# Three chained layers in one kernel: the tile's transposes cut into 64-row halves, and moved to other slots

## The reference, cut to what matters

```python
# x: (2, 4096, 192), weight_gen: (2, 4096, 8 heads, 7 taps)
w = softmax(weight_gen, axis=-1)
x1 = causal 7-tap convolution of x, head h (24 channels) weighted by w[:, :, h, :]
h = np.maximum(x1 @ w_in, 0.0)      # (8192, 192) @ (192, 2048)
x2 = h * h @ w_out                  # (8192, 2048) @ (2048, 192)
h = x2 @ w_in2
out = h * np.cos(h) @ w_out2
```

## Time and profile before

| | |
|---|---|
| median of 3 runs | 1298.72 us (1298.04 to 1299.22) |
| the profiled execution's own time | 1302.44 us |
| its span on the core | 1300.7 us |
| PE / DVE / ACT / POOL busy | 96% / 74% / 63% / 29% |
| mean granted clock of TensorE | 0.984 of full |

### The profile page before, as it was taken

How to read it: one execution, slowest core, us unless ns; L and a number is a source line. 1 busy time by engine, 2 the same in 40 slices (tenths; PEclk the granted TensorE clock), 3 DMA queues, 4 the chain that set the end, 5 groups by cost and what they waited for, 6 DMA issues and landing times.

```text
span 1300.7 us, 24802 instructions
## 1 busy us (share of the span) xinstructions
PE 1244.6 (96%) x9728; PEld 1076.9 (83%) x9728; DVE 965.2 (74%) x1439; ACT 822.8 (63%) x1487; POOL 372.4 (29%) x245
## 2 busy tenths in 40 slices
PE   3898999999999999999999999999999999999997
PEld 2555789898898979889897988989798998989755
DVE  7866777777877777787777778777777778777664
ACT  2477666666666666666666666666666666666654
POOL 3635560512406060330606042150604124000000
PEclk9887999999999999999999999999999999999998
DMA  5230000000001000000100000000100000000000
GB/s 164 63 104 12 32 31 1 14 31 14 31 1 43 2 14 31 14 31 2 44 1 14 31 13 32 13 31 1 39 6 14 31 13 1 2 13 2 13 1 24
DMA packets 13235, 31.72 MB, mean 24 GB/s; under 512 B 1348, under 2 KB 8770, under 8 KB 12992
## 3 DMA queue, kind: packets, MB, share of 16 engines
q1 hardware_dynamic: 13120, 30.14, 7.0%
HBM read 23.84 MB, written 6.29 MB: 23 GB/s over the span
## 4 chain that ended last, share of the span: by engine, by line
PE 82%; DVE 10%; issue 3%; ACT 3%; DMA 1%; SPq 0%; DVEq 0%; ACTq 0%
PE y L390 38%; PE h L390 38%; DVE h L814 2%; PE h L444 2%; DVE turns L797 1%; DVE h L793 1%; PE h L454 1%; DVE g_lo L826 1%; DVE g_lo L830 1%; ACT relu L655 1%; DVE y_part L811 1%; DVE xa_lo L818 1%; ACT turns L682 1%; ACT g_hi L705 1%; PE h L451 1%
## 5 line engine op out<-in xcount | busy, mean ns | idle before, releaser
L390 PE MATMUL y<-g_hi,wo 64*128 64x512 f32 x2820 | 557.2, 394 | 0.0
L390 PE MATMUL y<-g_lo,wo 64*128 64x512 f32 x1880 | 398.9, 391 | 0.0
L347 POOL TENSOR_TENSOR tap<-xc,gen 128x768 f32<-128x768 f32 x105 | 166.4, 1591 | 654.2 <-PE h L444 638.8
L390 PEld LDWEIGHTS y<-g_hi,wo 64*128 64x128 f32 x2820 | 300.7, 184 | 36.6 <-DVE xa_lo L818 3.3
L682 ACT ACTIVATE turns<-turns 128x512 f32<-128x512 f32 x256 | 161.8, 632 | 209.2 <-DVE turns L797 208.8
L814 DVE TENSOR_TENSOR h<-h,turns 128x512 f32<-128x512 f32 x256 | 179.1, 699 | 144.4 <-ACT turns L682 139.5
L793 DVE SCALAR_TENSOR_TENSOR h<-h,relu 128x512 f32<-128x512 f32 x256 | 178.7, 698 | 114.7 <-ACT relu L655 111.5
L655 ACT ACTIVATE relu<-h 128x512 f32<-128x512 f32 x256 | 152.9, 597 | 135.0 <-PE h L390 135.0
L390 PEld LDWEIGHTS y<-g_lo,wo 64*128 64x128 f32 x1880 | 203.7, 184 | 14.2
L390 PE MATMUL h<-xa_hi,wa_hi 64*128 64x512 f32 x940 | 201.8, 395 | 12.0 <-DVE g_lo L826 11.9
L390 PE MATMUL h<-xa_lo,wa_hi 64*128 64x512 f32 x940 | 200.9, 392 | 0.0
(11 more groups left out here) (90 smaller groups left out, 1167.8 us busy)
## 6 DMA issues: line engine op xcount, KB each, us to landing
xc<-in_x_dram SPq DMA_DIRECT2D x14, 960.0 KB
out_dram<-arena SPq DMA_DIRECT2D x16, 384.0 KB, 2.3
arena<-in_moe_w_out_dram SPq DMA_DIRECT2D x16, 192.0 KB, 2.8
arena<-in_moe_w_in_dram SPq DMA_DIRECT2D x16, 128.0 KB, 2.3
gen<-in_weight_gen_dram SPq DMA_DIRECT2D x1, 1568.0 KB, 9.4
arena<-in_moe_w_in_dram SPq DMA_DIRECT2D x16, 64.0 KB, 2.8
xc<-in_x_dram SPq DMA_DIRECT2D x1, 768.0 KB
xc<-in_x_dram SPq DMA_DIRECT2D x2, 283.5 KB
```

The costliest lines, as they stand in the source:

```text
L347: pool.tensor_tensor(tap[:, k % 2, :].rearrange("p (r g) -> p r g", g=GROUP), rows[k], wk, ALU.mult).then_inc(pool_step, 1)
L390: return pe.matmul(o, w[rows, :], x[rows, :], start=start, stop=stop)
```

## The change

1. Both turns are done as 64-row halves, `TOP` and `BOTTOM` in pairs, like all other matmuls: the x1 turn is 16 transposes of 64 rows by 128 columns into 64 columns of PSUM (both parts together), the output turn 12. The top half goes to one bank and the bottom half to another; `h1` and `h2` become four banks of one tensor, ordered so that the two banks that a slot does not use lie beside each other, and one ACT or DVE instruction can read both.
2. From tile 2 on (`t >= PEEL`) the x1 turn is whole in slot 8, the output turn whole in slot 12; in tiles 0 and 1 the x1 turn is whole in slot 13. A turn stands inside the a part of the downs (`a_first`), waits for `g_lo` of both layers of the slot before, and x1's is followed by two ACT copies and two DVE subtractions in a row.
3. In the slot behind the x1 turn, the downs' first halves are issued ahead of the ups; the ups wait for `x1_split`, both parts.
4. The two halves of `y2`'s d part are now added when they leave PSUM in slot 4: two ACT copies of 64x256 and two DVE additions of 64x256 in place of one DVE copy of 128x512. So `fold` and its matmuls are gone; the output turn has transposes alone, and ACT copies its result in two pieces.

```diff
-    TURN = SLOTS - 3
+    TURN = SLOTS // 2
...
+    def turn_at(t):
+        return TURN if t >= PEEL else SLOTS - 3
     def out_at(t):
-        return END_AT if isinstance(t, int) and t == TILES + 1 else TURN
+        return END_AT if t == TILES + 1 else TURN + 4
...
-        h1 = pb("h1")
-        h2 = pb("h2")
+        h = ctx.enter_context(nc.psum_tensor("h", [P, 4, TOK], F32))
+        h1 = [h[:, 0, :], h[:, 2, :]]
+        h2 = [h[:, 3, :], h[:, 1, :]]
...
+        def turn_banks(i):
+            return (0, 1) if i % 2 else (2, 3)
...
-            def turn_x1(bank, part):
+            def turn_x1(i, part):
                 for jj in range(JJ):
                     at = jj * DM + part * DA
-                    last = pe.transpose(h1[:, bank, jj * P:(jj + 1) * P], x1[:, at:at + P], ident[:, :])
+                    for side, bank in enumerate(turn_banks(i)):
+                        rows = slice(side * DD, (side + 1) * DD)
+                        o = part * TOK // 2 + jj * DD
+                        last = pe.transpose(h[:, bank, o:o + DD], x1[rows, at:at + P], ident[rows, rows])
                 return last
-            def turn_out(bank, q):
-                for jj in range(2):
-                    cols = slice((2 * q + jj) * P, (2 * q + jj + 1) * P)
-                    pe.transpose(h2[:, bank, jj * DM:jj * DM + DA], y2_sb[:, 0, cols], ident[:, :])
-                for jj in range(2):
-                    cols = slice((2 * q + jj) * P, (2 * q + jj + 1) * P)
-                    last = pe.matmul(h2[:, bank, jj * DM + DA:(jj + 1) * DM], y2_sb[:, 1, cols], fold[:, :],
-                                     start=True, stop=True)
+            def turn_out(i):
+                for jj in range(JJ + JJ // 2):
+                    for side, bank in enumerate(turn_banks(i)):
+                        rows = slice(side * DD, (side + 1) * DD)
+                        y = y2_a[rows, jj * P:(jj + 1) * P] if jj < JJ else y2_d[rows, (jj - JJ) * P:(jj - JJ + 1) * P]
+                        last = pe.transpose(h[:, bank, jj * DD:(jj + 1) * DD], y, ident[rows, rows])
                 return last
             def turns_of_slot(t, i, n, m):
-                if TURN <= i < TURN + 2 and tile_live(t + 1) and live(n):
+                x1_turn = i == turn_at(t) and tile_live(t + 1)
+                out_turn = i == out_at(t) and tile_live(t - 2)
+                if x1_turn or out_turn:
+                    pe.wait_ge(g1_ready, min(n, STEPS))
+                    if counted(m):
+                        pe.wait_ge(g2_ready, at_most(m))
+                if x1_turn:
                     pe.wait_ge(x1_ready, t + 1)
-                    pe.wait_ge(g1_ready, n)
-                    turn_x1((i + 1) % 2, i - TURN).then_inc(x1_turned, 1)
-                if out_at(t) <= i < out_at(t) + 2 and tile_live(t - 2):
-                    pe.wait_ge(g2_ready, at_most(m))
+                    for part in range(2):
+                        turn_x1(i, part).then_inc(x1_turned, 1)
+                if out_turn:
                     pe.wait_ge(y2_a_ready, t - 1)
                     pe.wait_ge(y2_d_ready, t - 1)
-                    turn_out((i - C2 + 1) % 2, i - out_at(t)).then_inc(out_turned, 1)
+                    turn_out(i).then_inc(out_turned, 1)
             def ups_of_slot(t, i, n, m):
...
-                    if TURN < i <= TURN + 2 and tile_live(t + 1):
-                        pe.wait_ge(x1_split, 2 * t + 2 + i - TURN)
+                    if i == turn_at(t) + 1 and tile_live(t + 1):
+                        pe.wait_ge(x1_split, 2 * t + 4)
+                    if i == out_at(t) + 1 and tile_live(t - 2):
+                        pe.wait_ge(out_ready, t - 1)
...
+                    pe.wait_ge(y1_d_done, n - D1)
...
+                def a_first():
+                    y1_free(t, i, y1_read)
+                    pe.wait_ge(down1_done, n - D1)
+                    down_a(down1, TOP, 0, start=True)
+                    y2_free(t, i, y2_a_ready)
+                    if counted(m - D2):
+                        pe.wait_ge(down2_done, m - D2)
+                    down_a(down2, BOTTOM, 0, start=True)
+                    down_a(down1, TOP, 1)
+                    down_a(down2, BOTTOM, 1)
+                    turns_of_slot(t, i, n, m)
+                    down_a(down1, TOP, 2).then_inc(y1_a_left, 1)
+                    down_a(down2, BOTTOM, 2).then_inc(y2_a_left, 1)
...
+                if i == turn_at(t) + 1 and tile_live(t + 1):
+                    d_first()
+                    a_first()
+                    ups_first()
+                    d_last()
+                    ups_last()
+                else:
+                    ups_first()
+                    d_first()
+                    ups_last()
+                    a_first()
+                    d_last()
+                a_last()
...
-                if TURN <= i < TURN + 2 and tile_live(t + 1) and live(n):
-                    part = i - TURN
-                    act.wait_ge(x1_turned, 2 * t + 3 + part)
-                    act.activation(x1_part(xa_hi, xd_hi, 1 - par, part), turned_x1(1 - b, part),
-                                   ACT.Copy).then_inc(x1_hi_ready, 1)
-                if out_at(t) <= i < out_at(t) + 2 and tile_live(t - 2):
-                    q = i - out_at(t)
-                    act.wait_ge(out_turned, 2 * (t - 2) + q + 1)
+                if i == turn_at(t) and tile_live(t + 1):
+                    act.wait_ge(x1_turned, 2 * t + 4)
+                    for part in range(2):
+                        act.activation(by_half(x1_high(1 - par, part)), turned_x1(i, part),
+                                       ACT.Copy).then_inc(x1_hi_ready, 1)
+                if i == out_at(t) and tile_live(t - 2):
+                    act.wait_ge(out_turned, t - 1)
                     if counted(t - 2 - par):
                         act.wait_ge(stored[par], (16 // 2) * (t - 2 - par))
-                    act.activation(out_sb[:, par, 2 * q:2 * q + 2, :],
-                                   h2[:, 1 - c, 0:2 * DM].rearrange("p (j d) -> p j d", j=2),
+                    act.activation(out_sb[:, par, :, 0:DA].rearrange("p j (h d) -> p j h d", h=2),
+                                   turned(i)[:, :, 0:JJ * DD].rearrange("p h (j d) -> p j h d", j=JJ), ACT.Copy)
+                    act.activation(out_sb[:, par, :, DA:DM].rearrange("p (h j) d -> p h j d", h=2),
+                                   turned(i)[:, :, JJ * DD:JJ * DD + JJ * DD // 2].rearrange("p h (j d) -> p h j d",
+                                                                                            d=DD),
                                    ACT.Copy).then_inc(out_ready, 1)
...
+                if i == Y2_AT and tile_live(t - 2):
+                    act.wait_ge(y2_d_done, SLOTS * (t - 1))
+                    if counted(t - 2):
+                        act.wait_ge(out_turned, t - 2)
+                    act.activation(y2_d[0:DD, :], y2[DD:P, 1, 0:TOK // 2], ACT.Copy)
+                    act.activation(y2_d[DD:P, :], y2[0:DD, 1, TOK // 2:TOK], ACT.Copy).then_inc(y2_part_ready, 1)
...
-                if TURN <= i < TURN + 2 and tile_live(t + 1) and live(n):
-                    part = i - TURN
-                    dve.wait_ge(x1_hi_ready, 2 * t + 3 + part)
-                    dve.tensor_tensor(x1_part(xa_lo, xd_lo, 1 - par, part), turned_x1(1 - b, part),
-                                      x1_part(xa_hi, xd_hi, 1 - par, part), ALU.subtract).then_inc(x1_split, 1)
+                if i == turn_at(t) and tile_live(t + 1):
+                    dve.wait_ge(x1_hi_ready, 2 * t + 4)
+                    for part in range(2):
+                        dve.tensor_tensor(by_half(x1_low(1 - par, part)), turned_x1(i, part),
+                                          by_half(x1_high(1 - par, part)), ALU.subtract).then_inc(x1_split, 1)
                 if i == Y2_AT and tile_live(t - 2):
-                    dve.wait_ge(down2_done, SLOTS * (t - 1))
-                    if counted(t - 2):
-                        dve.wait_ge(out_turned, 2 * (t - 2))
-                    dve.tensor_copy(y2_sb[:, 1, :], y2[:, 1, :]).then_inc(y2_d_ready, 1)
+                    dve.wait_ge(y2_part_ready, t - 1)
+                    for half in range(2):
+                        rows, cols = slice(half * DD, (half + 1) * DD), slice(half * TOK // 2, (half + 1) * TOK // 2)
+                        last = dve.tensor_tensor(y2_d[rows, :], y2[rows, 1, cols], y2_d[rows, :], ALU.add)
+                    last.then_inc(y2_d_ready, 1)
...
```

More of the change, by code:

```diff
@@ L586, in slot, with ups_first @@
-                down_d(down1, BOTTOM, 1, stop=True).then_inc(y1_d_done, 1)
-                pe.wait_ge(y2_a_left, pair)
-                down_a(down2, TOP, 0)
-                pe.wait_ge(y1_a_left, pair)
-                down_a(down1, BOTTOM, 0)
-                down_a(down2, TOP, 1)
-                down_a(down1, BOTTOM, 1)
-                down_a(down2, TOP, 2, stop=True).then_inc(down2_done, 1)
```

(36 more changed lines are left out.)

128 lines of the change are left out of this document (53 added, 75 removed).

## The result

The changed kernel takes **1269.35 us** (median of 4 runs, 1269.04 to 1269.59) beside 1298.40 for the kernel before (4 runs, 1298.04 to 1299.22): a ratio of 0.9775, with an interval of 0.9758 to 0.9792. It is faster by 29 us. The forecast was 1279 with a range from 1272, so the direction was right and the gain was larger than the range allowed. The profiled execution took 1269.21 us (span 1267.4); that of before was 1302.44.

What follows compares the result with a forecast made beforehand. PE, busy 96% of the span, was taken as the bound. Freeing L821 from POOL (11.3) and cheaper turns (8.2) sum to 19.5 us off 1298.7, giving 1279; its own range 1272 to 1286, the wider one 1272 to 1291.

Steps and rivals of the forecast that it cites:

- I take 0.11, since rows 10 show it for this very shape of load: PE's turns: a pair of 64-row transposes costs 0.11 us, bound by its weight loads; bounds 0.06 and 0.22.
- faster than 1272: PE's turns: pairs near 0.06 us give 9 us more, 1270; chance 0.04.
- x1's turn: On PE in slot 8: wait 0.13, first pair 0.05, eight pairs at 0.11, exit load 0.11; 1.17 us.
- the output's turn: On PE in slot 12: wait 0.13, first pair 0.05, six pairs at 0.11, exit load 0.11; 0.95 us.
- their 1.37 us of room: ACT's and DVE's spare time before PE needs their results two slots later; said to just hold slot 9's 1 us delay.
- Tiles 0 and 1 and the end ... I take as 0, give or take 1 us: Stretches where full and half matmuls mix: no gain or loss, give or take 1 us.
- 3.7 off: Whole kernel: the median of the runs lies 3.7 us below the profiled execution, giving 1298.7 as starting point.
- POOL's overlap: DVE's L821 before slot 3: POOL's convolution beside it costs 0.94 us a tile; freeing twelve tiles gains 11.3 us.
- Slot 9: Behind x1's turn: PE's ups wait about 0.1 us for `x1_split`, charged 0.10; 1.25 without the leading downs.
- The split of y2: Slot 4: adds about 0.5 us to ACT, nothing to DVE, covered by 1.37; without that cover 0.5 a tile.
- The convolution in slots 8 to 13 slows nothing: DVE beside POOL's moved convolution: its instructions read PSUM on one side, so no slowdown was charged.
- the transposes cost more on PE: PE's turns: row groups' loads take turns, 0.22 us a pair, 20 us more, 1299, no change; chance 0.08.

Runs made afterwards that it cites:

- experiment 4: The kernel before, unchanged, profiled once more: 1298.16 us, ratio 0.9999; its profiled execution took 1298.10.
- experiment 12: The changed kernel, unchanged, run again on another chip: 1266.95 us, ratio 0.9752; its profiled execution took 1265.21.
- experiment 5: The changed kernel with each turn's transposes reordered, one row group's behind the other's instead of in turn: 1271.07 us, ratio 0.9802.
- experiment 6: The changed kernel with every transpose of both turns done twice, into the same place: 1282.71 us, ratio 0.9877.
- experiment 1: The changed kernel with the two turns exchanged, x1's in slot 13 and the output's in slot 8: 1279.30 us, ratio 0.9842.
- experiment 3: The changed kernel with full 128x128 transposes in the turns, 8 for x1 and 6 for the output: 1280.15 us, ratio 0.9850.
- experiment 9: The changed kernel with unread extra matmuls ahead of the turns, 16 of 64 rows by 128 columns and 8 of 128 by 64: 1296.46 us.

## Why the prediction fell short

The profiled executions differ by 33.2, and the prediction worked out 19.5. By the same instruction of each tile (L821 and L885), the 33.2 lie as follows; "again" has the other pair of executions, experiments 4 and 12:

| stretch | measured | again | predicted |
|---|---|---|---|
| start, to tile 2's slot 1 | 1.9 | 3.5 | 0 |
| tile 2 | 1.35 | 1.4 | 0.63 |
| tiles 3 to 14 | 12 x 2.11 = 25.3 | 25.1 | 12 x 1.57 = 18.8 |
| tile 15 | 1.8 | 1.8 | 0 |
| end | 2.9 | 1.1 | 0 |

**The step that failed** is "I take 0.11, since rows 10 show it for this very shape of load", the price of a pair of half transposes. It is 0.062 (16 in 0.49 us). The lower bound in the prediction was 0.06, and the rival "faster than 1272" had named it, at 0.04, with 1270. 14 pairs x 0.05 is 0.70 a tile. That the two row groups' loads go beside each other was right; that a pair of loads is bound to 0.11 was not. The reading behind it was at fault: the earlier trace rows show two loads 0.11 apart in a stream where nothing needed them sooner, since two pairs of matmuls take 0.47 there. A spacing under no pressure is an upper bound of a price. In the changed kernel, PE's weight loads in slot 8 show what they can do:

```profile
502.94 0.61 PEld L470 LDWEIGHTS h<-ident,x 64*128 64x128 f32 x16 [0.32 <-issue]
503.43 0.34 PEld L414 LDWEIGHTS y<-g_hi,wo 64*128 64x128 f32 x4
```

Sixteen of the same shape in 0.49, and experiments 5 and 6 hold it fast: 0.06 from one to the next in a row group, with the other group's transposes beside them or not, and whatever their number. The loads of the earlier trace rows belong to plain matmuls, though, and whether those could also follow at 0.06 no run shows. A row for the bound from below was there too: 64 columns are an eighth of the 512 that take 0.233 for a pair.

Of x1's turn, 1.17 became 0.70: 0.40 from the pairs, the rest because the wait and the first load were charged one after the other (0.18) where they lie together (0.11). Of the output's turn, 0.95 became 0.77: 0.30 from the pairs, 0.04 from the exit, and 0.15 lost to its wait, which is 0.33 rather than 0.18. The prediction saw that slot 9's late ups delay ACT and DVE and let them be caught up within their 1.37 us of room; they are caught up, but only behind slot 12, and the turn there has no such room.

**"Tiles 0 and 1 and the end ... I take as 0, give or take 1 us"** was the second one: 1.9 at the start, 1.8 in tile 15 and 2.9 at the end, 6.6 together, and 6.4 in the other pair. At the end the last store is issued earlier: the timelines of before and after.

```profile
1297.89 0.33 SPq L293 DMA_DIRECT2D out_dram<-arena  x1
```

```profile
1264.66 0.33 SPq L320 DMA_DIRECT2D out_dram<-arena  x1
```

Of the 2.9, 1.3 lie in the last chain, from the start of the last `g_lo` (1291.45 and 1259.51) to this store: 6.4 to 5.15 us. The other 1.6 lie ahead of it, and most of that is the clock. Around the output turn of the last tile but one, the first execution of before had a granted clock of 0.83 (1266 to 1276 us), and that of the changed kernel 1.00 (1232 to 1242); in experiments 4 and 12 it is the other way round, and the end differs by 1.1 instead of 2.9. Experiment 4, at 1.00 there, reaches the last `g_lo` only 0.5 later than the changed kernel's first execution. So of the 6.6 only the 1.8 of tile 15 is the same in both pairs. Tiles 0, 1 and 15 and the end got the cheaper turns as well, and the prediction had multiplied by 13 only. That reading is from the traces; no experiment took these stretches apart, and what shortens the start stays open.

The median moved by 29.05, not 33.2. The prediction took 3.7 off for the profiled execution of before being above its median. That of after isn't (1269.21 and 1269.35): its four runs lie within 0.6 us of the profiled one, whose start was at the lower clock. On the third chip the medians are 32.0 apart (1298.99 and 1266.95). So that 1270, the prediction's sum with a pair at 0.06, comes so near the measured 1269.35 is in part luck: its sum would be 28.5 then, where the profiled executions are 33.2 apart.

**What was right.** POOL's overlap: L885 at 0.69 from tile 3 on and slot 3 starting 0.12 late (said: 0.15), confirmed by experiment 1. The Trainium skill, SBUF — State Buffer, section SBUF: two separate sides, agrees in every run that has both cases: 1.78 and 1.88 with POOL beside it, 0.69 without. Slot 9: 0.10 of waiting, as said, and 0.08 behind it, and 1.26 for the 1.25 without the lead. The split of y2 is free; slots 4 and 5 keep 4.43. The convolution in slots 8 to 13 slows nothing: L865 takes 0.67 at 505.44 with POOL at work. The count in the rival "the transposes cost more on PE" is off: a tile of the kernel before has 12 full transposes and four plain matmuls, recorded as eight, and not 16 and eight; no sum uses it.

The Trainium skill, TensorE: Matmul & The Clock Gate, has rules on both sides of the failed step. Its section LDWEIGHTS (loading the stationary operand) says that a load takes its columns / 1.2 GHz and that fewer rows don't shorten it: an estimate of 0.107 us here. The full-row matmuls agree (0.11 apart in experiments 3 and 9); the half transposes don't, at 0.062 within one row group, so there the measurement decides. Its section "Wait — 56ns, not 53.3ns?" gives a matmul's columns / 2.4 GHz + 2.5 ns: estimates of 0.029 for 64 and 0.056 for 128 columns. The averages over both row groups, 0.031 and 0.057, come near them, but the trace does not bear the rule out: within one group a start follows the last at 0.062 and 0.11, about twice as late.

## What to carry to other kernels

Before a move of work is costed, find which engine's stretch it drags along: here the turn's slot set POOL's, and POOL's set the length of a subtraction on DVE three slots later. A price read from a stream in which nothing pressed is an upper bound, not the price. What a change does to the common tile it does to the first and the last as well, and work taken apart into more slots pays its gap in each of them.

## What the runs showed of the hardware

- Transposes of 64 rows into 64 columns start 0.06 us apart in their row group, and the two groups run side by side: 16 take 0.49, 32 take 1.00. Full transposes (128 rows, 128 columns) start 0.11 apart, and so do plain matmuls of 128 rows and 64 columns.
- Plain matmuls of 64 rows take 0.11 a pair for 128 columns and 0.233 for 512.
- PE kept the program's order within a row group, but not between the two: in experiment 5 an upper matmul started ahead of three lower transposes that stand before it. Changing the order of issue did not take the groups apart.
- The two profiled executions of each kernel differ by 4 us, with another granted clock in the start (0.55 to 0.59 or 1.00 at 110 to 120 us) and in the end (0.83 or 1.00 around the last output turn but one), and with the changed kernel's tile distances equal to 0.01 us. In a comparison of 1% or less it is the tile distance that tells.
